# An mLSTM + two-MLP kernel: POOL's attention work a chunk earlier, a reordered opening, matmuls of ones in it

## The reference

```
# attention: 2 x 8 heads, 768 steps, head size 40
m_new = max(f + m, i);  C = exp(f + m - m_new) * C + exp(i - m_new) * v k^T ;  n likewise with k
y = sigmoid(o) * (C q) / max(|n q|, 1)
# MLP over 1536 tokens of 320, hidden 2048
h = x @ w_in ;  x2 = max(0.01 * h, h) @ w_out
# experts: logits = x2 @ w_gate, argmax, capacity 384
out[token] = gate * (relu(x2 @ w1[e]) @ w2[e])
```

## Time and profile before

| what | us |
|---|---|
| median of three executions | 525.8 |
| lowest, highest | 520.43, 528.17 |
| the profiled execution, its own time | 524.6 |
| its span from first to last instruction | 522.9 |
| PE busy (82% of the span) | 426.9 |
| DVE, ACT, POOL busy | 269.5, 217.3, 182.2 |
| mean granted clock of PE, 1 being full speed | 0.901 |

### The profile page before, as it was taken

One profiled execution on the slowest core, in us unless ns is written; L12 is line 12 of the kernel. 1 busy time (PEld: TensorE's weight loads), 2 busy tenths in 40 slices (PEclk: granted clock), 3 DMA queues, 4 the chain that ended last, 5 costly groups with the idle time before them and its releaser, 6 DMA issues.

```text
span 522.9 us, 7854 instructions
## 1 busy us (share of the span) xinstructions
PE 426.9 (82%) x2905; PEld 407.1 (78%) x2905; DVE 269.5 (52%) x556; ACT 217.3 (42%) x477; POOL 182.2 (35%) x185
## 2 busy tenths in 40 slices
...
GB/s 219 375 282 252 49 60 108 53 55 104 51 88 22 107 46 1 1 2 1 266 1 122 0 242 161 102 93 178 59 223 0 59 236 306 268 21 4 3 1 53
DMA packets 17848, 55.88 MB, mean 107 GB/s; under 512 B 4248, under 2 KB 7514, under 8 KB 17792
## 3 DMA queue, kind: packets, MB, share of 16 engines
...
...
## 4 chain that ended last, share of the span: by engine, by line
PE 38%; DVE 8%; issue 7%; ACT 4%; DMA 3%; POOL 1%; ACTq 0%; POOLq 0%; DVEq 0%
PE bank L1208 15%; PE bank L1195 5%; PE bank L1196 4%; PE bank L1197 4%; DVE w1l L791 3%; PE bank L1199 2%; PE bank L1198 2%; DMA xd<-x 2%; PE bank L1279 1%; ACT w1h L583 1%; PE bank L1238 1%; DVE gl L987 1%; DVE g L979 1%; DMA xg<-xd,idg 1%; ACT gh L716 1%
## 5 line engine op out<-in xcount | busy, mean ns | idle before, releaser
L496 POOL TENSOR_TENSOR w2l<-w2r,w2h 128x640 fp32r<-128x640 f32 x32 | 50.1, 1569 | 117.0 <-ACT w2h L588 116.8
L1005 DVE SCALAR_TENSOR_TENSOR gl<-bank,gh 128x384 fp32r<-128x384 f32 x64 | 35.6, 556 | 99.4 <-ACT gh L716 98.7
L696 ACT ACTIVATE tt<-bank 128x384 f32<-128x384 f32 x64 | 31.3, 489 | 99.4 <-PE bank L1199 99.4
L1195 PE MATMUL bank<-xeh,w1h 128*128 128x256 f32 (+1 forms) x128 | 43.6, 341 | 33.8 <-issue 26.8
L716 ACT ACTIVATE gh<-bank 128x384 fp32r<-128x384 f32 x64 | 31.5, 493 | 93.6 <-PE bank L1208 89.2
L1208 PE MATMUL bank<-woh,gh 128*128 128x320 f32 x192 | 62.6, 326 | 5.8 <-DVE gl L987 5.7
L979 DVE TENSOR_TENSOR g<-bank,tt 128x384 f32<-128x384 f32 x64 | 35.4, 553 | 55.3 <-ACT tt L696 55.2
L1208 PE MATMUL bank<-woh,gl 128*128 128x320 f32 x192 | 59.8, 311 | 0.0
L1208 PE MATMUL bank<-wol,gh 128*128 128x320 f32 x192 | 59.8, 311 | 0.0
L1195 PEld LDWEIGHTS bank<-xeh,w1h 128*128 128x128 f32 x128 | 25.8, 202 | 40.2 <-issue 33.8
L702 ACT ACTIVATE gh<-g 128x384 fp32r<-128x384 f32 x64 | 33.4, 522 | 47.7 <-DVE g L979 47.7
...
## 6 DMA issues: line engine op xcount, KB each, us to landing
...
```

The costliest lines, as they stand in the source:

```text
L496: gp.tensor_tensor(lo, raw, hi.bitcast(F32), ALU.subtract).then_inc(s_lo2, 1)
L696: a.activation(tt[m % 2][:], ps_h[m % 2][:, 0:TM], ACT.Copy, scale=0.01).then_inc(s_t, 1)
L1005: ve.scalar_tensor_tensor(gl[m % 2][:], ps_h[m % 2][:, 0:TM], 0.0, gh[m % 2][:].bitcast(F32), ALU.max, ALU.subtract).then_inc(s_gl, 1)
L1195: mm(hb, wh[:, f, kt, :], x_hi[:, kt, ts], start=kt == 0, stop=False)
```

## The change

- `scale_v(n+1)` and `decay(n+1)` are issued on POOL in chunk n's places SC and P1; they were in chunk n+1's place E0. `one_plus` leaves POOL: ACT adds the one itself, an Identity activation with bias 1.0 that waits for `exp_o`.
- Chunk 2's arguments come through DRAM too (`NARG = 2`; it was 3): `args(2)` leaves PE, `spread_gates(2)` enters SP's queue behind chunk 2's loads, and `gsc` is stored by ACT's queue instead of SP's. Weights 0 and 1 are now issued behind `spread_gates(2)`.
- q and k of a chunk come in one transfer of 104 partitions (416 KB, with the rows between the halves as zeros) instead of two of 40 (160 KB each). The three memsets of that padding leave DVE, and SP no longer waits for them. The two memsets of PSUM banks (0.48 us each) move from DVE to ACT.
- The order of the opening changes on DVE, PE and POOL, and PE issues matmuls of ones there: 7 at the start, 8 before and 6 behind the last transposes, each 128x128 by 512 columns in bf16, into banks that nobody reads.
- The maximum of `den` with 1 becomes a tensor-tensor operation with a tile of ones, `one8`.

```diff
+    NARG = 2
             def spread_gates(n):
-                if n == SOLO:
+                if n == NARG:
                     sp.wait_ge(s_gsc, 16)
-                sp.wait_ge(s_P, 2 * (n - 2))
+                else:
+                    sp.wait_ge(s_P, 2 * (n - 2))
...
             load_chunk(2)
+            spread_gates(2)
             load_wi(0)
             load_wo(0)
-            sp.wait_ge(s_gg, 1)
-            sp.dma_start(gsc, gg[:]).then_inc(s_gsc, 16)
...
-                if k == E0:
-                    one_plus(n)
-                    scale_v(n)
-                    decay(n)
+                if k == SC and n + 1 < NCH:
+                    scale_v(n + 1)
                 elif k == INTER and n + 1 < NCH:
                     cut_args(n + 1)
+                elif k == P1 and n + 1 < NCH:
+                    decay(n + 1)
...
                 a.activation(eo[n % 2][:], on[n % 3], ACT.Exp, scale=-1.0).then_inc(s_eo, 1)
+                act.wait_ge(s_eo, n + 1)
+                a.activation(eo[n % 2][:], eo[n % 2][:], ACT.Identity, bias=1.0).then_inc(s_eo1, 1)
...
+            act.wait_ge(s_const, 3)
+            for b in (ps_o, bank[7]):
+                last = a.activation(b[:], onesb[:, 0:1].broadcast_to([P, 512]), ACT.Copy, scale=0.0)
+            last.then_inc(s_zps, 1)
             exp_o(0)
+            act.wait_ge(s_gg, 1)
+            act.dma_start(gsc, gg[:]).then_inc(s_gsc, 16)
...
-                link(ve.tensor_scalar(den[:], den[:], 1.0, None, ALU.max))
+                link(ve.tensor_tensor(den[:], den[:], one8[:], ALU.max))
...
             new_state(0)
-            reciprocal_o(1)
-            head_sums(0)
             probs(1, 0)
             probs(1, 1)
+            head_sums(0)
             scale_inter(1)
+            reciprocal_o(1)
             new_state(1)
             probs(2, 0)
             probs(2, 1)
             head_sums(1)
+            scale_inter(2)
             x_low(0)
-            scale_inter(2)
             reciprocal_o(2)
+            head_sums(2)
             new_state(2)
-            head_sums(2)
...
+            def keep_warm(b, count):
+                for _ in range(count):
+                    mm(b[:].rearrange("p (a t) -> p a t", a=4), onesb[:],
+                       onesb[:].unsqueeze(1).broadcast_to([P, 4, P]), start=True, stop=True)
-            pe.wait_ge(s_const, 2)
+            pe.wait_ge(s_const, 3)
+            keep_warm(bank[6], 7)
+            pe.wait_ge(s_zps, 1)
```

74 lines of the change are left out of this document (33 added, 41 removed).

## The result

The changed kernel took 505.10 us, the median of three executions (504.60, 505.10, 508.77); the kernel before took 526.98 beside it (four executions, 520.43 to 528.47). The ratio is 0.9641, with a 95% interval of 0.9535 to 0.9747: faster. The profiled execution took 504.60 us, its span is 502.9 us against 522.9, and its mean granted clock 0.915 against 0.901.

A forecast was written before the change was run, and what follows sets the result against it. PE was taken as the bound in the MLP, losing time to `vs` waits and clock drops, and a chain through all engines before 41 us. 524.6 - 7.4 - 10 - 5 = 502.2, median put at 503 us, range 493 to 515.

The forecast's parts named there:

- Term 2: Between 50 and 256 us: PE's waits for POOL's `vs` go, 10 us won, bounds 6 and 11.5.
- Term 3: Clock drops behind PE's idle stretches in the MLP: 5 us of 8.4 won back, bounds 0 and 8.4.
- Term 1: Opening up to `acc_step(0)`: 43.1 to 43.4 us against 50.80, 7.4 us won, bounds 4.5 and 9.7.
- The ones in front end at 6.3 and don't move the gates: Start of PE: transposes about 6.3 for 6.06; `scores(0)` at full speed saves 1.0 us, exponents at 11.0.
- `ee(2)` lands at 17.3: Chunk 2's transfers through DRAM: 3 us for `gsc`, 5.3 for `ee`, landing at 17.3; bounds 15 and 28 after the cut.
- The `probs` of chunk 1 follow the cuts: Opening, POOL then DVE: cuts end at 19.6, 1.8 us later than before; then `probs`, with `t1` at 22.2.
- `hs(2)` at 31.6, MLP at 38.0: Late opening: chunk 2's `hs` at 31.6 against 35.25, MLP start at 38.0, 3.1 us sooner.
- Step 0 at full speed: First MLP step, with ones on both sides: 1.45 us at full speed, `h_step(0)` ending at 39.5.
- `gl(0)` 3.1 us behind `h_step(0)` and then 0.5: MLP step 0: `gl(0)` comes 3.1 us behind `h_step(0)` plus 0.5 for ACT's added instruction; `acc_step(0)` at 43.1 to 43.4.
- the opening wins nothing: Rival, chance 0.20: MLP starts at 41, winning only the 2.8 us wait and part of step 0; 509 us.
- The `den` edit: DVE's maximum of `den` with 1: costed at 0, still held by POOL; 1 us in all if free.
- Work behind 304 us is untouched: Everything behind the MLP's last step, the experts included: no change, 0 us.

The follow-up runs named there:

- e2_before_ahead: The kernel before, with only `scale_v` and `decay` issued a chunk ahead on POOL: 507.48 us, ratio 0.966.
- e1_no_ahead: The changed kernel with `scale_v` and `decay` put back into place E0 of their own chunk: 511.72 us, ratio 0.976.
- e8_plus_on_pool: The changed kernel with the addition of one to exp(-o) back on POOL in its old place: 501.59 us, ratio 0.957.
- e11_cut_first_only: The changed kernel with POOL's cut of chunk 1's exponents ahead of its cut of chunk 2's arguments, all ones kept: 501.53 us, ratio 0.955.
- e4_no_first_ones: The changed kernel without the first 7 matmuls of ones; the 8 and 6 stay: 499.62 us, ratio 0.953.
- e6_cut_first: The changed kernel without its first 7 ones and with POOL cutting chunk 1's exponents ahead of chunk 2's arguments: 497.88 us, ratio 0.951.
- e3_no_ones: The changed kernel without all 21 matmuls of ones: 503.41 us, ratio 0.961.
- e5_ones_late: The changed kernel without its first 7 ones, but with 7 more ones at the end of the MLP stage: 502.56 us, ratio 0.956.

## Why the prediction was right, and where it was off

**Term 2, the waits for `vs`: right.** Predicted 10 us. The windows over the middle, of the kernel before and of the one after:

```profile
55.50:304.00 248.50, 230.29 (x1565) 221.84 (x1565) 150.38 (x312) 104.84 (x240) 56.90 (x63) 0.97 0.18 60
```

```profile
51.20:282.00 230.80, 222.00 (x1566) 214.31 (x1566) 151.59 (x313) 108.15 (x248) 48.42 (x54) 1.00 0.21 68
```

PE's idle time there is 248.5 - 230.3 = 18.2 us before and 230.8 - 222.0 = 8.8 after: 9.4 us won. e2_before_ahead shows that POOL's work a chunk ahead does this alone; e1_no_ahead shows that without it 4.6 us of them stay, so the rest of the change takes the others away as well. The 0.5 to 0.7 us left for two chunks came as `DVE gl` and `DVE x` waits of up to 0.8. What the prediction costed at nothing and was not nothing is the addition on ACT: "the two meet" was said of `gl(4)`, and 1.9 us in all show they did not quite (e8_plus_on_pool).

**Term 3, the clock: right mechanism, mis-sized.** PE's busy time for the same instructions fell from 230.3 to 222.0, 8.3 us, of which I took 5; with the edit of term 2 alone it fell to 223.4. The bound of 8.4 was the sum over four windows, 60 of the 248 us, so it is chance that the whole stretch comes out at it. In the changed kernel up to 240 us no wait over 0.9 us is left, and the clock is 1.00 in the whole middle. The waits before `scores` (1.9 us, twice, at most 0.9) remained and no drop followed. I had discounted for them without a row that showed a drop behind so short a stop.

**Term 1, the opening: mis-sized, 4.4 for 7.4.** Its steps one by one.
- *The ones in front end at 6.3 and don't move the gates.* Right: they end at 6.3, and the transposes of the gates start at 6.12 for 6.3. What failed is that they make `scores(0)` run at full speed. It took 2.08 us as before, and the exponents start at 12.16 for 11.0. e8_plus_on_pool, with the same ones, had `scores(0)` in 1.16 us, as had e1_no_ahead and e11_cut_first_only, so this is not settled by the ones. It didn't matter: POOL's wait ate it (e4_no_first_ones).
- *`ee(2)` lands at 17.3.* It landed at 18.6. Rows of the kernel after, `gsc` (L628) and the ten `ee` (L349):

```profile
DMA to landing us min/median/max: 5.5/5.5/5.5
...
DMA to landing us min/median/max: 4.1/6.3/12.2
```

  `gsc` took 5.5 us for my 3, `ee(2)` about 4.2 for my 5.3. On ACT's queue it is quicker than the 9.4 of the earlier trace rows, as by the rule of turns between queue rows that the prediction quoted from the Trainium skill (DMA: Bandwidth & Descriptors, Queues, rings and completion order); the trace agrees in direction, though the change also holds the weights back, and 5.5 us for 48 KB says that the loads in front were not passed for nothing.
- *The `probs` of chunk 1 follow the cuts.* The cuts ended at 20.9 for 19.6, `t1` at 23.7 for 22.2. This is the step that failed, and the failure is not the 1.3 us. I took the order on POOL as given and priced it as "1.8 us later than before". Turning it round gave 4.5 us at the first MLP matmul with the first ones (e11_cut_first_only) and 6.9 without (e6_cut_first against e4_no_first_ones). What I had missed is the work queued behind on two more engines: the reciprocal of 2.14 us, which could have run in the wait, and PE's three pieces of chunk 1 (`state`, `intra`, `inter`), which fell behind the drop of the clock.
- *`hs(2)` at 31.6, MLP at 38.0.* 34.70 and 41.07. The late cut accounts for 1.2 of these 3.1 us: DVE was through with chunk 2's `probs` at 27.6 for 26.4. The other 1.9 came behind, where the prediction had said "waits a little for PE": DVE waited 1.22 us for `intra(1)` and 0.66 us for ACT's `x_hi(0)`. PE ran at half speed there (granted 0.50 from 22 to 36 us, behind its stop of 3.51 us): `inter(2)` took 1.98 us where it had taken 1.02, `state(2)` 1.66 for 0.96. The prediction priced the clock of step 0 and of the MLP, and not of this stretch. In e11_cut_first_only, with `t1` 5.1 us sooner and no such stop, `hs(2)` comes 6.1 us sooner and the MLP 4.5. Behind `hs(2)` the terms held: 6.4 us to the MLP and 5.3 more to `acc_step(0)`, for 6.4 and 5.4. But the load that `vs` of chunk 3 needs, ahead of `y` of chunk 2 on POOL, was in no term of mine; the kernel with that order turned round is the fastest.
- *Step 0 at full speed.* Right, and shown by e3_no_ones: 1.3 us of the 4.4. The rest of the gain is the `vs` wait of 2.83 us.
- *`gl(0)` 3.1 us behind `h_step(0)` and then 0.5.* Right: `h_step(0)` ends at 42.7 and `acc_step(0)` starts at 46.4, 3.7 us later, with exp(-o), the addition and the exponents in front of `gh(0)`.

So the opening did what the rival "the opening wins nothing" said (PE starts the MLP at 41, wins the 2.8 us wait and part of step 0), with 0.20 of the chance, and the total was held by a larger term 3. That the sum, 502.2, came within 2.4 us of the 504.6 of the profiled execution is luck in this: an opening 3.0 us too good, a middle 2.8 us too modest, and 2.1 us behind that were in no term. That rival's 509 used a clock term of 3 us. With the measured 8.3 it gives 524.6 - 3 - 10 - 8.3 = 503.3, and the profiled execution took 504.6.

**The `den` edit: right, 0.** After, by line:

```profile
L857 DVE TENSOR_TENSOR den<-den,one x12: 661/674/729, 22.4 to 222.7; 128x8 f32<-128x8 f32 x12
```

674 ns against 682. It was held by POOL's product as before. By the rule of the Trainium skill (GPSIMD Engine Reference, Specifications) on two SBUF inputs it had to be; this trace agrees. Where POOL stood still, in the opening of e11_cut_first_only at 17.8 us, the same instruction took 0.17 us, so it is free there; whether the old form would have too, no run shows.

**"Work behind 304 us is untouched": wrong by 2.1 us.** No edit touches it, but PE's program has 21 ones more and 8 transposes fewer in front of it. Without the first 7 ones it is 6.6 us shorter (e4_no_first_ones), and 7 ones put in at another place bring back 3.9 of these (e5_ones_late), with a stall of PE named "issue". The prediction had named this stretch as a place where the gain could go. Why 8 transposes fewer and 14 ones more leave it 4.5 us shorter than before (214.3 for 218.8) stays open.

**The other rivals.** ACT did not become the bound (PE's waits for `gl` are 2.2 us in all), but on a small scale it was right: 1.9 us. POOL's queue did hold things up, by 4.5 to 6.9 us and not by the 22 that the slower case needed.
